# First loads split into column halves and four fold-weight subtractions placed at steps 2, 3, 7 and 9 of a fused FFT and MLP kernel

## The reference

```python
def _attn_ref(x):                       # x: (2, 3008, 256)
    X = np.fft.fft(x, axis=1)
    X = np.fft.fft(X, axis=2)
    return X.real.astype(np.float32)

def _moe_ref(x, w_in, w_out):           # 6016 tokens, 256 -> 2048 -> 256
    h = x @ w_in
    g = h * (1.0 / (1.0 + np.exp(-h)))
    return (g @ w_out).astype(np.float32)

def _moe2_ref(x, w_in, w_out, alpha):
    h = x @ w_in
    g = np.maximum(h, 0.0) + alpha * np.minimum(h, 0.0)
    return (g @ w_out).astype(np.float32)
```

## Time and profile before

| | us |
|---|---|
| median of 3 runs | 934.04 (933.5 to 935.79) |
| the profiled execution, its whole time | 933.09 |
| its span in the trace | 931.2 |
| PE busy | 923.3 (99%) |
| PE loading weights (beside the matmuls) | 757.2 |
| DVE busy | 635.2 |
| GpSimd busy | 594.4 |
| ACT busy | 551.6 |

### The profile page before, as it was taken

One profiled execution on the slowest core, in us unless ns is written; L12 is line 12 of the kernel. 1 busy time (PEld: TensorE's weight loads), 2 busy tenths in 40 slices (PEclk: granted clock), 3 DMA queues, 4 the chain that ended last, 5 costly groups with the idle time before them and its releaser, 6 DMA issues.

```text
span 931.2 us, 11837 instructions
## 1 busy us (share of the span) xinstructions
PE 923.3 (99%) x4034; PEld 757.2 (81%) x4034; DVE 635.2 (68%) x967; ACT 551.6 (59%) x858; POOL 594.4 (64%) x408
## 2 busy tenths in 40 slices
PE   9999999999999999999999999999999999999998
PEld 4588887788888888888888888888888888888886
DVE  6879996455545545544877777777777777778774
ACT  4575654567667656676665565465555555555544
POOL 0496555259959859676697476566747756664443
PEclk9999999999999999999999999999999999999999
DMA  9512100020020120100300200020020002001001
GB/s 361 222 56 68 45 1 1 1 67 23 13 78 23 55 80 1 45 1 1 124 11 1 71 20 1 0 89 1 1 88 1 1 1 89 1 1 44 1 1 45
DMA packets 19826, 40.35 MB, mean 43 GB/s; under 512 B 1803, under 2 KB 15669, under 8 KB 18741
## 3 DMA queue, kind: packets, MB, share of 16 engines
q1 hardware_dynamic: 18980, 39.05, 11.9%
q10 hardware_dynamic: 688, 0.52, 0.2%
q0 software_dynamic: 96, 0.02, 0.0%
HBM read 27.22 MB, written 12.37 MB: 43 GB/s over the span
## 4 chain that ended last, share of the span: by engine, by line
PE 94%; DVE 2%; POOL 1%; DMA 1%; ACT 1%; issue 0%; SPq 0%; DVEq 0%; ACTq 0%; POOLq 0%
PE ps L354 12%; PE ps L352 12%; PE ps L353 12%; PE ps L668 9%; PE ps L671 9%; PE ps L667 9%; PE ps L613 9%; PE ps L609 9%; PE ps L610 9%; DMA x_tile<-x_tiles 1%; PE ps L556 1%; POOL gl L1313 1%; PE ps L541 1%; PE ps L537 1%; POOL wo L1248 0%
## 5 line engine op out<-in xcount | busy, mean ns | idle before, releaser
L1335 POOL TENSOR_TENSOR gl<-g,gh 128x502 fp32r<-128x502 f32 x192 | 224.8, 1178 | 175.3 <-ACT gh L857 175.3
L1313 POOL TENSOR_TENSOR gl<-g_sb,gh 128x1004 fp32r<-128x1004 f32 x96 | 210.3, 2190 | 121.2 <-ACT g_sb L814 119.2
L851 ACT ACTIVATE g<-ps 128x502 f32<-128x502 f32 x192 | 111.9, 591 | 110.3 <-DVE ps L1196 105.3
L1148 DVE SCALAR_TENSOR_TENSOR h_sb<-n_all,a,v_sb 128x502 f32<-128x502 f32 x96 | 83.1, 865 | 135.1 <-ACT v_sb L876 135.0
L1203 DVE SCALAR_TENSOR_TENSOR g<-g,less_alpha,ps 128x502 f32<-128x502 f32 x192 | 132.6, 732 | 31.9 <-ACT g L851 31.8
L609 PE MATMUL ps<-gh,wo 128*128 128x502 f32 x384 | 148.8, 388 | 0.3
L610 PE MATMUL ps<-gh,wo 128*128 128x502 f32 x384 | 147.9, 385 | 0.0
L667 PE MATMUL ps<-gh,wo 128*128 128x502 f32 x382 | 147.3, 386 | 0.0
L668 PE MATMUL ps<-gh,wo 128*128 128x502 f32 x382 | 147.3, 386 | 0.0
L857 ACT CAST gh<-g 128x502 fp32r<-128x502 f32 x192 | 113.0, 614 | 40.3 <-DVE g L1203 38.6
L876 ACT COPY v_sb<-ps 128x502 f32<-128x502 f32 x96 | 55.6, 580 | 122.5 <-PE ps L354 118.4
(11 more groups left out here) (132 smaller groups left out, 1618.4 us busy)
## 6 DMA issues: line engine op xcount, KB each, us to landing
x_tile<-x_tiles SPq DMA_DIRECT2D x6, 1024.0 KB, 13.5
x_rows<-x SPq DMA_DIRECT2D x6, 1004.0 KB, 5.9
out_t<-out_sb SPq DMA_DIRECT2D x11, 502.0 KB, 3.2
x_raw_b<-x_rows SPq DMA_DIRECT2D x18, 251.0 KB, 4.0
stage<-moe_w_out SPq DMA_DIRECT2D x16, 256.0 KB, 4.5
n_parts<-n_rows SPq DMA_DIRECT2D x5, 502.0 KB, 3.7
stage<-moe_w_in SPq DMA_DIRECT2D x8, 256.0 KB, 5.0
w_sb<-moe_w_in SPq DMA_DIRECT2D x3, 512.0 KB, 7.8
```

Source lines behind the costliest of these rows:

```text
L851: act.activation(g4[:, k, :], product_bank(u, TILE_IN[k]), ACT.Relu, scale=-1.0).then_inc(relu_done, 1)
L1313: pool.tensor_tensor(gl[g % 2][:, :, :], g_sb[g % 2][:, :, :], gh[g % 2][:, :, :].bitcast(F32), ALU.subtract).then_inc(gl_done, 1)
L1335: pool.tensor_tensor(gl4[:, k, :], g4[:, k, :], gh4[:, k, :].bitcast(F32), ALU.subtract).then_inc(gl_done, 1)
```

## The change

- `w_sb`'s first half block (128x512) comes in two loads of 256 columns, with a semaphore each. PE does the first products of jobs 0 and 1 on these halves (`feature_first`), both jobs' first half, then both jobs' second half, and then `feature` adds the rest.
- The table `mt` is laid out in DRAM so that each half of it has 256 contiguous floats in a partition's row. Before, it was two rows of 128.
- x tiles 0 and 1 come in two halves each (columns 0 to 511 with 1024 to 1535, then the rest), each of which is what one `fold_sum` reads. The order of the loads is x0 first half, x0 second half, w 2, x1 first half, w 3, x1 second half; it was x0, w 2, w 3, x1.
- `IDLE` goes from 4 to 3.
- DVE's `ab_low(4)` and `ab_low(5)` move from after step 0 to after steps 2 and 3, ahead of nothing else in these steps' lists.
- GpSimd's `ab_low(6)` and `ab_low(7)` move from ahead of `split_lo(0)` to after `gl` of steps 7 and 9. Its wait for `t1_lo` goes, and it now waits for `w_done` (L1148 of step 0) ahead of `split_lo(0)`.

```diff
--- before.py
+++ after.py
@@ -38,7 +38,10 @@
 SLOTS = 4
 A_JOBS = [(1, 0), (0, 0), (1, 1), (0, 1), (1, 2), (0, 2), (1, 3), (0, 3)]
 FOLD_AFTER = [*range(4, 16), *range(18, 27)]
-IDLE = 4
+IDLE = 3
+
+AB_DVE_AFTER = {2: 4, 3: 5}
+AB_POOL_AFTER = {7: 6, 9: 7}
 JOB_AFTER = {1: "n", 28: "t1p", 29: "t1q", 30: "t2", 31: "t3"}
 
 
@@ -109,7 +112,7 @@
         ab_whole = at("ab_whole", AB_AT, [P, 2, 2, FF], F32)[:, :, 1, :]
         wo2 = at("wo2", AB_AT, [P, NF, 2, D], F32R)
 
-        mt = at("mt", OPA_AT, [P, 2, FEATW], F32)
+        mt = at("mt", OPA_AT, [P, 2, 2, P], F32)
         w_sb = at("w_sb", OPA_AT + 2048, [P, 2, FF], F32)
         n_all0 = at("n_all0", OPA_AT, [P, N], F32)
         v_sb = at("v_sb", OPA_AT + 2016, [P, N], F32)
@@ -176,7 +179,8 @@
         stage_lo = sem("stage_lo")
         mt_in = [sem(f"mt_in{m}") for m in range(2)]
         w_in = [sem(f"w_in{i}") for i in range(4)]
-        w0_in = sem("w0_in")
+        w0_in = [sem(f"w0_in{i}") for i in range(2)]
+        xa_in = [sem(f"xa_in{t}") for t in range(2)]
         t1_in = [sem(f"t1_in{q}") for q in range(QT)]
         t2_in = sem("t2_in")
         t3_in = sem("t3_in")
@@ -408,6 +412,13 @@
             def load_x(t):
                 sp.dma_start(xbuf[t][:, :], x_tiles[t]).then_inc(x_in[t], 16)
 
+            def load_x_half(t, i):
+
+
+                sp.dma_start(xbuf[t][:, :].rearrange("p (r i d) -> p r i d", r=2, i=2)[:, :, i, :],
+                             x_tiles[t].rearrange("p (r i d) -> p r i d", r=2, i=2)[:, :, i, :]
+                             ).then_inc(x_in[t] if i else xa_in[t], 16)
+
             def load_t1(q):
                 sp.dma_start(t1_sb[:, 2 * q:2 * q + 2, :], t1[q]).then_inc(t1_in[q], 16)
 
@@ -422,14 +433,17 @@
                     sp.dma_start(n_rows[first:last, i * N:(i + 1) * N].rearrange("(a c) t -> a c t", a=1),
                                  pq[0:1, first:last, 2 + i, :].bitcast(F32)).then_inc(n_out, 16)
 
-            sp.dma_start(w_sb[:, 0, 0:512], moe_w_in[0:P, 0:512]).then_inc(w0_in, 16)
+            for i in range(2):
+                sp.dma_start(w_sb[:, 0, 256 * i:256 * i + 256], moe_w_in[0:P, 256 * i:256 * i + 256]).then_inc(w0_in[i], 16)
             sp.dma_start(w_sb[:, 1, 0:512], moe_w_in[P:2 * P, 0:512]).then_inc(w_in[0], 16)
             load_w(1)
             sp.dma_start(x_half_sb[:, :, :, :], x_half).then_inc(half_in, 16)
-            load_x(0)
+            load_x_half(0, 0)
+            load_x_half(0, 1)
             load_w(2)
+            load_x_half(1, 0)
             load_w(3)
-            load_x(1)
+            load_x_half(1, 1)
             load_t1(0)
             load_x(2)
             load_t1(1)
@@ -502,16 +516,22 @@
             def feature(k):
 
                 m, fb = A_JOBS[k]
-                if k < 2:
-                    pe.wait_ge(mt_in[m], 16)
-                for j in range(2):
-                    if fb == 0 and j == 0:
-                        pe.wait_ge(w0_in, 16)
-                    else:
-                        pe.wait_ge(w_in[fb], 16)
-                    ins = pe.matmul(ps[:, k, :], mt[:, j, m * P:(m + 1) * P],
+                pe.wait_ge(w_in[fb], 16)
+                for j in range(1 if fb == 0 else 0, 2):
+                    ins = pe.matmul(ps[:, k, :], mt[:, m, j, :],
                                     w_sb[:, j, fb * 512:(fb + 1) * 512], start=j == 0, stop=j == 1)
                 ins.then_inc(a_pe, 1)
+
+            def feature_first(k, i):
+
+
+                m, fb = A_JOBS[k]
+                if i == 0:
+                    pe.wait_ge(mt_in[m], 16)
+                if k == 0:
+                    pe.wait_ge(w0_in[i], 16)
+                cols = slice(256 * i, 256 * i + 256)
+                pe.matmul(ps[:, k, cols], mt[:, m, 0, :], w_sb[:, 0, cols], start=i == 0, stop=False)
 
             def two_a():
 
@@ -675,6 +695,9 @@
             pe.wait_ge(idle_done, 1)
             for _ in range(IDLE):
                 pe.matmul(ps[:, 7, 0:224], pq_raw[:, 0, 0, 0:P], pq_raw[:, 0, 0, 0:224], start=True, stop=True)
+            for i in range(2):
+                for k in range(2):
+                    feature_first(k, i)
             for k in range(len(A_JOBS)):
                 feature(k)
 
@@ -781,7 +804,7 @@
                 ins.then_inc(t23_hi, 1)
 
             for m in (1, 0):
-                act.dma_start(mt[:, :, m * P:(m + 1) * P], feat_dft[:, :, m * P:(m + 1) * P]).then_inc(mt_in[m], 16)
+                act.dma_start(mt[:, m, :, :], feat_dft[m]).then_inc(mt_in[m], 16)
             act.wait_ge(spare_done, 1)
             act.activation(spare[:, 0:1], spare[:, 1:2], ACT.Silu)
             for k, (m, fb) in enumerate(A_JOBS):
@@ -957,7 +980,9 @@
 
             def fold_sum(t, i):
 
-                if i == 0:
+                if i == 0 and t < 2:
+                    dve.wait_ge(xa_in[t], 16)
+                elif i == 0 or t < 2:
                     dve.wait_ge(x_in[t], 16)
                 X = xbuf[t]
                 up = X[:, 1024 + 512 * i:1536 + 512 * i]
@@ -1170,9 +1195,8 @@
                     t1_late_low(1, former[2])
                 elif former == "t3":
                     n_hold_low()
-                if g == 0:
-                    ab_low(4)
-                    ab_low(5)
+                if g in AB_DVE_AFTER:
+                    ab_low(AB_DVE_AFTER[g])
                 if g in FOLD_AFTER:
                     i = FOLD_AFTER.index(g)
                     fold_piece(QT + i // 7, i % 7)
@@ -1303,9 +1327,8 @@
             pool.wait_ge(ab_lo, 2)
             ab_low(2)
             ab_low(3)
-            pool.wait_ge(t1_lo, 2)
-            ab_low(6)
-            ab_low(7)
+
+            pool.wait_ge(w_done, 1)
             split_lo(0)
             for g in range(STEPS1):
                 pool.wait_ge(gh_done, g + 1)
@@ -1314,6 +1337,8 @@
                                    ALU.subtract).then_inc(gl_done, 1)
                 if g < WO2_ITEM - 1:
                     split_lo(g + 1)
+                if g in AB_POOL_AFTER:
+                    ab_low(AB_POOL_AFTER[g])
                 c, f = divmod(g, NF)
                 if f == NF // 2 and c + 1 < NC1:
                     add_n(c + 1)
@@ -1414,7 +1439,7 @@
     t1 = t1.reshape(QT, 2, P, T1W).transpose(0, 2, 1, 3)
     t1[1] = t1[1].reshape(2, P // 2, 2, T1W).transpose(2, 1, 0, 3).reshape(P, 2, T1W)
     t2, t3 = (t.transpose(1, 0, 2) for t in t23)
-    return [np.ascontiguousarray(t, dtype=np.float32) for t in (feat.reshape(2, P, FEATW).transpose(1, 0, 2), t1, t2, t3)]
+    return [np.ascontiguousarray(t, dtype=np.float32) for t in (feat.reshape(2, P, 2, P).transpose(2, 1, 0, 3), t1, t2, t3)]
 
 
 def token_columns():
```

## The result

The changed kernel takes 937.83 us (median of eight, 936.73 the lowest) against 934.09 before, a ratio of 1.0033 with a 95% interval of 1.0022 to 1.0045. A second measurement beside the experiments gave 937.69 against 933.79, 1.0044 (1.0027 to 1.0060). By the two ratios the change costs 3.1 and 4.1 us. PE is busy 925.4 of 935.3 us there.

The account below looks back on a forecast made before the run. PE was taken as the bound, busy 923.3 of 931.2 us. 0.18 + 2.63 = +2.8 us on 933.09 gives 935.9, stated as 936.8 because the median lay 0.95 above that execution; range 932.8 to 937.8.

Parts of the forecast that it names:

- the cascade: Steps 7 to 14: L1148(11) waits behind gl(10), gl(11) comes late, first1(14) 2.63 us later; 936.8 us, chance 0.42.
- s: Start of the kernel: x tile halves let DVE's fold_sum begin sooner, 0.35 us gained, between 0 and 0.65.
- The lows: Moved ab_low(4) to (7): first1(2) 0.75 us earlier besides s, but gl(7) ends 0.53 later less s.
- The path to the cascade: Steps 7 to 11: GpSimd goes first 1.63 us after gl(7) ends; if DVE were first, 3.2 us in all.
- T: Time counted from the end of gl(7), which is T = 0; gl(10) was to end at 11.80.
- The front: Weights and x tiles in halves, one idle matmul fewer: PE begins 0.3 to 0.8 us earlier, DVE's fold gains s.
- PE has only to be ready by then: Front: transforms1(1) at 21.65 waits for DVE's fold of tile 1, so PE's earlier start gains nothing; 0.5 us in hand.
- C: Rival, front: with three idle matmuls PE's clock may rise later, costing 1.0 us at 3 us, 935.5; chance 0.07.
- A: Rival, step 11: L1148(11) gets in before gl(10), no cascade, +0.5 us, 934.5; chance 0.36.
- B: Rival, faster: GpSimd wins the tie at gl(1) and later, period 4.21 instead of 4.34, 933.2 us; chance 0.10.
- D: Rival, front: x tile halves land later than 15.56, say by 0.5 us, shifting everything, 935.4; chance 0.05.
- The line of 0.3%: A measurement tells about 0.3% (2.8 us) from no change; slower 0.22, same 0.72, faster 0.06.

Follow-up runs that it names:

- the two fronts with IDLE = 3 alone: Kernel before plus the change without ab_low moves and w_done wait: 934.62 against 933.79; the same with whole x tiles: 934.69 against 934.05.
- the lows alone: Kernel before with only the ab_low moves and the wait for w_done: 937.16 us against 933.79, ratio 1.0035.
- The two parts apart: Kernel before with only ab_low(4), (5) moved: 934.70 against 934.23; with only ab_low(6), (7) moved and the w_done wait: 936.47 against 934.23.
- two pairs of kernels: IDLE 4 against 3: changed kernel 937.00 against 937.69; change without ab_low moves and w_done wait 933.75 against 934.62.

## Why the prediction was right, point by point

The forecast was the cascade, at 936.8 us with a range up to 937.8, and 937.83 was measured, at the range's very end. Its parts, from the second traced execution:

| step of the prediction | forecast | measured |
|---|---|---|
| first1(2), from first1(0) | 0.75 earlier | 0.74 earlier (7.49, 8.23) |
| gl(1) ends, from first1(0) | 15.30, as before | 15.35 |
| gl(7) ends, from first1(0) | 0.53 later than 40.80 | 0.58 later (41.38) |
| first1(14) after gl(7)'s end | 19.77 | 19.74 |
| front, s | 0.35 earlier | later; 0.8 and 0.6 us by the two fronts with IDLE = 3 alone, neither clear of no change |

*The lows* were right in mechanism and size. 0.53 and 2.63 make 3.16; the lows alone show 3.19 in the trace and 3.3 in time. What was won by taking ab_low(6) and (7) off the start (0.74 at first1(2)) went exactly where it was said to go: gl(1) is bound by ACT's chain and by the ab_low(4) ahead of it. The two parts apart give 0.96 and 2.32, by traces.

*The path to the cascade* was partly the other one. At the end of gl(7) plus 1.63 I let GpSimd go first, because ab_low is 0.03 shorter than wo; DVE was first (L1030 at 78.03, gl(8) at 78.04), for which I had 3.2 us in all. gl(8) and gl(9) then ended 0.58 and 0.19 later than on my path (at T + 4.34 and 7.94 for 3.76 and 7.75), but gl(10), all the same, ended at T + 11.74 for 11.80, and everything behind hangs on that end. gl(10) beat L1173(11) by 0.18 us, where I had 0.16 on the one path and 0.45 on the other. So 2.6 us came out where 3.2 stood for the path that was taken, and the agreement of first1(14) within 0.03 is partly luck; that L1173 would lose was worked out.

*The front* failed. Two of its steps did. "PE has only to be ready by then", with 0.5 us in hand and C as a rival at 0.07: behind three idle matmuls the first feature matmuls run at the lower level, to 5.9 at the earliest and 10.6 us at the latest in five traces (to 4.2 to 6.3 in the nine with four), so transforms1(0) begins at 19.4 to 21.6 in place of 18.7 to 19.7 with four, and the 0.5 us in hand are gone in four of the five. That was no rival but what happens. Its price is some 0.7 to 1.1 us by two pairs of kernels, each less than its interval can settle, and 0.6 by the means of first1(0). And s came from one landing: in the traced execution before, tile 0 and tile 1 landed at 9.77 and 14.89, the earliest of all; the whole tile 0 landed between 9.77 and 11.08 in the traces with whole tiles, and first1(0) stood between 34.00 and 35.33 in the nine traces with IDLE = 4. 34.00 was the earliest of them. The term s was mis-sized: its ground, that the second half might land when the whole tile had, did not hold, since it landed 0.60 later on the mean, and nothing is left of the 0.35. Most of what the forecast of 936.8 lacks is this: about +0.7 us from the front where it had -0.35.

*Rivals.* A (no cascade, 934.5) fell. B (faster) fell. C came true on top of the forecast, not on top of A: its sign, feature matmuls 0.85 apart (0.43 for halves of 256 columns), stands in four of the five traces, and it was put at up to 1.0 us where the pairs show 0.7 to 1.1. D's late landing was seen in all six traces with halves (15.87 to 16.50, past its 15.56), but seven of the eight whole tiles came after 14.89 too, at 15.45 to 16.21, so that only the 0.60 between the means is the halves'.

*The line of 0.3%.* I had given 0.22 to a loss beyond it; with the front at +0.7 instead of -0.35 the sum is 0.53 + 2.63 + 0.7 = 3.9 us, where the two measurements have 3.1 and 4.1 by their ratios and 3.7 and 3.9 by their medians. The ratios of 1.0033 and 1.0044 lie beyond the line, both with an interval that takes it in.

## What to carry to other kernels

Where two engines exclude each other, a move of work is priced by which operation stands in front of which, not by its length: write down, for the steps around the new place, which waiting operation runs next, and follow the loser's consumers to the bound engine. A short operation whose result gates a whole step (here L1148) must not come up just behind a long one of the other engine; here leads of 0.02 and 0.18 us decided over steps 1.8 and 2.0 us longer. And a gain at the start of a pipeline is worth only what is left of it at the first stage that another chain bounds: of the 0.74 us that the wait for w_done wins at first1(2), 0.34 are left at first1(14).

## What the runs showed of the hardware that was not expected

- The clock of TensorE. PE was busy with idle matmuls from 1.19 to 3.80 (three) or to about 4.5 (four); the feature matmuls began at 4.04 to 4.70 behind three and at 4.29 to 5.38 behind four, as their loads landed. At the lower level (1.2 GHz) 256 columns stand 0.43 apart and 512 columns 0.85, at the upper (2.4 GHz) 0.22 and 0.43. With three, the change from one spacing to the other comes between 5.9 and 10.6 us (5.9, 7.6, 8.9, 9.4 and 10.6 in the five traces), with four between 4.2 and 6.3 in the nine; in one with four it came at 5.2, while PE stood idle for 0.83 us. So one idle matmul (0.74 us) more came with the upper level 3.5 us sooner on the mean, and when it comes differs by up to 4.7 us among executions that start alike. The view of the granted clock reads 1.00 all through; the record behind it has no entry before one of full clock, and that entry begins where the spacing changes (5.91 and 10.62 us in the earliest and the latest with three). For the first microseconds the level has to be read from the spacing or from that entry.
- The races repeat. The order at 86 us was the same in the four traces in which the lows were all moved and the quarter stood in step 10, and in the one with ab_low(6) and (7) alone, though first1(0) differed by up to 0.5 us; gl(10) led by 0.17 to 0.20 in all five. Even the 0.01 to 0.02 us by which L1030 was ahead of gl(8) came out the same five times. That the operations are tied to each other's ends, so that such a lead is kept, is my reading; no run tests it.
